# Attention and two feed-forward blocks on one core: two output places for lone heads, and the orders of small loads, exponentials, turns and fill pairs

## The reference, cut to what matters

```python
scores = scale * q @ k.T                       # (B, H, 576, 576)
cum = np.cumsum(np.maximum(s, 0), axis=-1)
bias = -(cum[..., :, None] - cum[..., None, :])
scores = np.where(causal, -1e9, scores + np.minimum(bias, 0.0))
scores -= scores.max(-1, keepdims=True)
attn = np.exp(scores); attn /= attn.sum(-1, keepdims=True) + 1e-9
x = heads_side_by_side(attn @ v)               # (B, 576, 512)
h = np.maximum(x @ w_in, 0)                    # 512 -> 1024
conv_out = conv over positions, 3 taps, per channel
x = (h * sigmoid(conv_out)) @ w_out            # 1024 -> 512
u = x + (x.T @ U @ V).T                        # mixes the 576 positions, rank 32
out = u + np.maximum(u @ w_ch1, 0) @ w_ch2     # 512 -> 2048 -> 512
```

## Time and profile before

| what | value |
|---|---|
| median of 3 runs | 921.22 us (920.56 to 921.58) |
| the profiled execution | 922.75 us |
| its span, first to last instruction | 921.0 us |
| PE busy | 873.2 us (95%) |
| DVE busy | 483.6 us (53%) |
| ACT busy | 373.2 us (41%) |
| POOL busy | 41.6 us (5%) |
| mean granted clock of TensorE | 0.98 |

### The profile page before, as it was taken

How to read it: one execution, slowest core, us unless ns; L and a number is a source line. 1 busy time by engine, 2 the same in 40 slices (tenths; PEclk the granted TensorE clock), 3 DMA queues, 4 the chain that set the end, 5 groups by cost and what they waited for, 6 DMA issues and landing times.

```text
span 921.0 us, 15633 instructions
## 1 busy us (share of the span) xinstructions
PE 873.2 (95%) x6184; PEld 831.9 (90%) x6184; DVE 483.6 (53%) x992; ACT 373.2 (41%) x709; POOL 41.6 (5%) x85
## 2 busy tenths in 40 slices
PE   4888898989999999999999999999999999999998
PEld 3676898879999999898999999988999999999998
DVE  6778794554448843554335871356225670442222
ACT  2667584654425634544233553444121431321110
POOL 3020000000000000000000000000000000000000
PEclk9979899989999999999999999999999999999999
DMA  7679356634764356435544453444243434355441
GB/s 161 167 211 308 111 149 204 217 79 149 239 200 173 131 190 200 153 115 198 174 153 144 144 170 113 166 128 163 92 151 140 181 138 177 144 189 182 145 177 52
DMA packets 63628, 149.14 MB, mean 162 GB/s; under 512 B 29514, under 2 KB 43850, under 8 KB 51012
## 3 DMA queue, kind: packets, MB, share of 16 engines
q1 hardware_dynamic: 61252, 144.50, 47.8%
q0 software_dynamic: 2304, 3.65, 1.7%
HBM read 117.97 MB, written 30.09 MB: 161 GB/s over the span
## 4 chain that ended last, share of the span: by engine, by line
PE 82%; DVE 8%; issue 4%; ACT 4%; DMA 1%; POOL 0%; DVEq 0%; ACTq 0%; POOLq 0%
PE psum L1170 22%; PE psum L1172 21%; PE psum L1171 21%; PE psum L1151 7%; PE psum L1098 3%; PE psum L1130 2%; PE psum L1128 2%; DVE psum L875 1%; PE psum L1135 1%; DVE work L942 1%; DMA spread_out<-few_scratch 1%; PE psum L1111 1%; ACT qc L675 1%; PE psum L1225 1%; DVE sums L895 1%
## 5 line engine op out<-in xcount | busy, mean ns | idle before, releaser
L1170 PE MATMUL psum<-uu_hl,ring 128*128 128x288 f32 x512 | 156.6, 306 | 7.6 <-DVE u_acc L997 2.9
L1170 PE MATMUL psum<-r_hl,ring 128*128 128x288 f32 x512 | 154.5, 302 | 1.9 <-DVE u_acc L997 1.1
L1172 PE MATMUL psum<-uu_hl,ring 128*128 128x288 f32 x512 | 152.8, 298 | 0.0
L1171 PE MATMUL psum<-uu_hl,ring 128*128 128x288 f32 x512 | 152.6, 298 | 0.0
L1172 PE MATMUL psum<-r_hl,ring 128*128 128x288 f32 x512 | 151.1, 295 | 0.0
L1171 PE MATMUL psum<-r_hl,ring 128*128 128x288 f32 x512 | 151.0, 295 | 0.0
L985 DVE SCALAR_TENSOR_TENSOR r_hl<-psum,r_hl 128x288 fp32r<-128x288 f32 x128 | 58.4, 457 | 133.9 <-ACT r_hl L773 133.9
L773 ACT ACTIVATE r_hl<-psum 128x288 fp32r<-128x288 f32 x128 | 52.4, 410 | 183.3 <-PE psum L1172 183.2
L1151 PE MATMUL psum<-probs,va 128*128 128x320 f32 (+4 forms) x448 | 117.4, 383 | 6.2 <-ACT probs L681 6.2
L875 DVE CUSTOM_DVE_ANT_0 psum<-psum,key_late 128x512 f32<-128x512 f32 (+4 forms) x160 | 84.7, 564 | 60.6 <-PE psum L1098 60.1
L1170 PEld LDWEIGHTS psum<-uu_hl,ring 128*128 128x128 f32 x512 | 97.8, 191 | 11.2 <-DVE u_acc L997 4.2
(11 more groups left out here) (104 smaller groups left out, 1654.1 us busy)
## 6 DMA issues: line engine op xcount, KB each, us to landing
ring<-w_scratch SPq DMA_DIRECT2D x74, 1024.0 KB, 4.8
w_scratch<-ring SPq DMA_DIRECT2D x24, 1024.0 KB, 6.1
kq_raw<-in_kq_t SPq DMA_DIRECT2D x64, 288.0 KB, 5.2
stage<-in_w_ch SPq DMA_DIRECT2D x16, 512.0 KB, 5.4
out_t<-u_acc SPq DMA_DIRECT2D x16, 288.0 KB, 3.9
va<-in_v SPq DMA_DIRECT2D x32, 128.0 KB, 2.4
spread_out<-few_scratch POOLq DMA_DIRECT2D x24, 144.0 KB, 4.3
stage<-in_w_out SPq DMA_DIRECT2D x4, 512.0 KB, 6.8
```

The lines of the kernel that those rows point to most:

```text
L1170: pe.matmul(o, hi, m_hi, start=start, stop=False)
L1171: pe.matmul(o, hi, m_lo, start=False, stop=False)
L1172: return pe.matmul(o, lo, m_hi, start=False, stop=stop)
```

## The change

- Output place: a head of body 0 with an even number gets its output four banks up (`out_at`), in banks 6 and 7; its values wait for the eviction of the head before the last one only. In body 0 the eviction of a head stands behind the next head's exponentials 0 and 1 on ACT (the last of the eight heads keeps its place).
- The small loads are issued in steps (0, 4), (1, 4) and (2, 2). POOL's memset writes the border columns of `hid` only, 4 instead of 1156.
- The turn stands in step 3 in all bodies; in bodies 1 to 3 it is behind the values of the step.
- `order`: the fill pair in the middle of "wi" goes, and where there are late pairs, one stands behind the split. With the spread by costs this moves other items by a step or two.
- ACT: after the last item of a step, the high part of a gated block and the making of a weight block (`follow`) stand behind the next attention step instead of ahead of it.
- DVE: x_low in bodies 1 to 3 stands behind the items of its step. `invert_few` of body 0 moves from step 3 to step 4.

```diff
@@ -224,6 +224,10 @@
         O0 = 3 * BANK - SPLIT
...
+        def out_at(n):
...
+            return O0 + 4 * BANK * (n < H and n % 2 == 0)
         MX = 4 * BANK
@@ -247,9 +251,10 @@
         UV_AT = (3, 2)
+        SMALL_AT = {(0, 4): 0, (1, 4): 1, (2, 2): 2}
         MAXIMA = [{0: (0, 1), 1: (2,)}, {0: (0,), 1: (1,), 2: (2,)}]
-        TURN = [3, 4]
+        TURN = [3, 3]
@@ -283,8 +288,6 @@
                 seq.extend(pair("wi", b, f))
-                if f == FT // 2:
-                    fill(1)
             fill(1)
@@ -298,12 +301,14 @@
                 fill_between(*([("mix", b, 0, d, half) for d in range(KT)] for half in range(2)))
+                seq.append(("split", b, 0, KT - 1, 0))
+                fill(1)
             else:
...
                     seq.extend(pair("mix", b, d))
-            seq.append(("split", b, 0, KT - 1, 0))
+                seq.append(("split", b, 0, KT - 1, 0))
             assert not late
@@ -427,6 +432,11 @@
+        LAST_OF_STEP = {items[-1] for plan in PLAN.values() for items in plan if items}
+        STEPS = [(a, h, g) for a in PLAN for h, g in ATT_STEPS]
+        STEP_BEFORE = dict(zip(STEPS[1:], [items for plan in PLAN.values() for items in plan]))
...
         X_SPLIT = [{(5, 0): 0, (7, 0): 1}, {(3, 4): 0, (5, 4): 1, (7, 4): 2}]
@@ -556,8 +566,8 @@
                     attention_step(0, h, g)
-                    if g == 4 and h < 3:
-                        load_small(h)
+                    if (h, g) in SMALL_AT:
+                        load_small(SMALL_AT[h, g])
                     if g == 1 and h - 1 in WEIGHTS_HEADS[:-1]:
@@ -640,7 +650,7 @@
                             pool.wait_ge(s_uvl, 2)
-                            pool.memset(hid[:, :, :], 0.0).then_inc(s_hid, 1)
+                            pool.memset(hid[:, :, 0:S + 2:S + 1], 0.0).then_inc(s_hid, 1)
@@ -683,6 +693,7 @@
                     o, sm = D * (h % 2), D * (1 - h % 2)
+                    out = out_at(n)
                     mm_pv.wait(act, n)
@@ -690,13 +701,13 @@
                     if h // 2 < NPAIR - 1:
-                        act.activation(sums[sm:sm + 1, h // 2 % 2, :], psf[sm:sm + 1, O0:O0 + S], ACT.Identity, bias=EPS)\
+                        act.activation(sums[sm:sm + 1, h // 2 % 2, :], psf[sm:sm + 1, out:out + S], ACT.Identity, bias=EPS)\
                            .then_inc(evict.sem, 1)
                     else:
-                        act.activation(sums[o:o + D, h // 2 % 2, :], psf[sm:sm + D, O0:O0 + S], ACT.Identity, bias=EPS)\
+                        act.activation(sums[o:o + D, h // 2 % 2, :], psf[sm:sm + D, out:out + S], ACT.Identity, bias=EPS)\
                            .then_inc(evict.sem, 1)
                     xl_done.wait(act, m - NPAIR)
-                    act.activation(x_raw[o:o + D, h // 2, :], psf[o:o + D, O0:O0 + S], ACT.Copy).then_inc(evict.sem, 1)
+                    act.activation(x_raw[o:o + D, h // 2, :], psf[o:o + D, out:out + S], ACT.Copy).then_inc(evict.sem, 1)
@@ -710,10 +721,12 @@
                         prepare_queries(a, h + 2)
-                    if g == 4:
+                    if g == 4 and (a or h == H - 1):
                         evict_head(a, h)
...
                         exponentials(a, h, c)
+                    if g == 0 and h and not a:
+                        evict_head(a, h - 1)
                     if (h, g) in X_SPLIT[a > 0]:
@@ -782,12 +795,26 @@
+                def follow(item):
+                    kind, b, unit, i, half = item
+                    if kind == "wi" and half and i:
+                        y_high(b, i - 1)
+                    for of, q in REFILL.get(item, ()):
+                        if made(of, q):
+                            weights_high(q)
...
+                def body_step(a, h, g):
+                    attention_step(a, h, g)
...
+                    if STEP_BEFORE.get((a, h, g)):
+                        follow(STEP_BEFORE[a, h, g][-1])
...
                 def ffn_step(item):
...
                         hidden(b, i, half)
-                        if i:
-                            y_high(b, i - 1) if half else gate(b, i - 1)
+                        if i and not half:
+                            gate(b, i - 1)
                     if kind == "gated":
@@ -800,9 +827,8 @@
                         hidden2(b, unit, i, half)
-                    for of, q in REFILL.get(item, ()):
-                        if made(of, q):
-                            weights_high(q)
+                    if item not in LAST_OF_STEP:
+                        follow(item)
@@ -813,7 +839,8 @@
                 act.wait_ge(s_hid, 1)
-                bodies(attention_step, ffn_step)
+                bodies(body_step, ffn_step)
+                follow(PLAN[B - 1][-1][-1])
                 for x, item in enumerate(END):
@@ -906,19 +933,19 @@
                         maxima(a, h + 1, r)
-                    if a and (h, g) in X_SPLIT[1]:
-                        x_low(a, X_SPLIT[1][h, g])
                     for pair in X_SPLIT_LAST[min(a, 2)].get((h, g), ()):
...
                         x_low(a, X_SPLIT[0][h, 0])
+                    if a and (h, g) in X_SPLIT[1]:
+                        x_low(a, X_SPLIT[1][h, g])
                     if g == 3 and not a:
...
                         query_low(a, h + 2)
-                    if g == 3 and h in (2, 4, 6):
+                    if g == 4 - (a > 0) and h in (2, 4, 6):
                         invert_few(a, h // 2 - 1)
@@ -1142,13 +1169,14 @@
                         v_in[i].wait(pe, a * NPAIR + h // 2)
-                        evict.wait(pe, n - 1)
+                        evict.wait(pe, max(n - 2, -1) if n < H else n - 1)
+                    out = out_at(n)
                     at = WIDTH[c]
...
                         first = (c, t) in ((0, 1), (3, 0))
-                        mm = pe.matmul(psf[:, O0 + i0:O0 + i1], va[i][:, t, :], probs[:, c % 2, at:at + w],
+                        mm = pe.matmul(psf[:, out + i0:out + i1], va[i][:, t, :], probs[:, c % 2, at:at + w],
                                        start=first, stop=True, skip_group_check=True)
@@ -1156,10 +1184,12 @@
                         scores(a, h, 1)
-                    if g == TURN[a > 0]:
+                    if g == TURN[0] and not a:
                         max_transpose(a, h + 1)
...
                         values(a, h, g - 1)
+                    if g == TURN[1] and a:
+                        max_transpose(a, h + 1)
                     if g in (1, 2):
```

## The result

The changed kernel takes **914.73 us** (median of 8 runs, 912.62 to 916.73) beside 921.31 us for the kernel before on the same chip (8 runs, 916.50 to 923.58): a ratio of 0.9934, 95% interval 0.9912 to 0.9956. It is faster, but by 6.6 us, where the sum had 17.7, and it lies above the upper end of the range, 913.

The account below looks back on a forecast made before the run. TensorE, busy 873.2 of 921.0 us, was taken as the bound, so only its idle and low-clock time could be won. Terms summed to -17.7 us: 903.5 on the median's scale, forecast 904, 8-in-10 range 898 to 913.

Parts of the forecast that it names:

- Lone heads, 0: Body 0's heads: PE's 0.42 us wait for exponentials only moves to DVE, so 0 us; bounds 2.9 won, 0.4 lost.
- Small loads, -5.0: Body 0 near 48 us: sooner small loads and a shorter memset end PE's stall and low clock, -5.0 us.
- rival 3: Small loads land no sooner, behind SP's queue and a 1 MB store: 909 us; chance 0.08.
- Transition, +0.5: Start of body 1: PE idles 3.4 us ahead of the sooner turn, products follow at low clock; +0.5 us.
- Body 1, gated part, +1.0: Exponentials' 2.37 us wait moves to DVE; low part and sooner turn wait some 0.65 us each; +1.0 us.
- Body 1, mixing part, -5.3: Waits of 1.57 and 1.64 us go, exponentials wait 1.5 us; idle -1.7, clock -3.6; bounds 0 and -6.1.
- So idle falls by 1.7: Body 1's mix: two waits go, about 1.5 us for exponentials comes instead, so 1.7 us less idle.
- stays up: Body 1's mix: full clock from 198.6 to 208.6 saves 4.4 us, less 0.8 us of wait: -3.6 us.
- Body 2, -3.8: Pair covers 1.9 us idle, low clock 1.7 and x_low's wait 1.2 go, gated part gives back 1.0: -3.8 us.
- Body 3, -5.1: Pair covers 1.9 us idle, low clock 3.0 and x_low's wait 1.2 go, gated part gives back 1.0: -5.1 us.
- The rule weighed in the prediction: Frequent small idles between groups of matmuls can also make the clock go down and up; by it rival 1 happens.
- rival 1: Several small waits stay in each mixing part and the clock falls all the same: 912 us; chance 0.20.

Follow-up runs that it names:

- one reordering by itself: Kernel before with nothing but x_low behind the step's items on DVE in bodies 1 to 3: 914.08 us, ratio 0.9913.
- the best kernel: Changed kernel with turn at step 4, y's high part at once, only the weights' high part behind the next attention step: 907.74 us, ratio 0.9846.

## Why the prediction was wrong, point by point

By the table (and with the 0.05 and 0.73 us of "up" counted to the mix) the parts changed as follows, from before to after:

| part | forecast | profile: idle + clock |
|---|---|---|
| body 0, up to the wait ahead of the turn | -5.0 | -1.95 + 1.6 = -0.35 |
| start and gated part of body 1 | +1.5 | +1.2 - 1.5 = -0.3 |
| mix of body 1 | -5.3 | +0.6 - 1.2 = -0.6 |
| body 2 | -3.8 | -0.1 - 1.7 = -1.8 |
| body 3 | -5.1 | -2.3 - 3.1 = -5.4 |

So two terms fell short by 4.7 us each, the small loads and the mix of body 1, and body 2 by 2.0. That the gated part does not show among them is the clock of this one execution and a shorter first wait; what it cost is told by the runs without turn and deferral.

**Lone heads, 0: right.** There the prediction followed the gain round the whole cycle of a head, to DVE; the terms that failed followed it one step.

**Small loads, -5.0: mis-sized**, 2 to 4 us where it shows, about 0 in the changed kernel. The step that failed is "Their four issues took 41.93 to 45.8, 3.9 us, so they end by 42.3": they began at 39.53, took 5.5 us and ended at 45.03. I counted the instructions that move, but put them behind a store and a load that are issued at 37.19 and 37.82, and gave them the durations they had had in another place. That is rival 3's mechanism, SyncE's queue and the 1 MB store ahead; its price was 5.0 us, as the term's. With the loads ahead of the store this step is mended and the time is still the same within the interval, so it is not all that the term had wrong: the next wait, for the spread sums, and the clock took the rest. The memset's part was right: the cast beside it takes 0.45 us instead of 1.40.

**Transition, +0.5: right in place.** The wait of 2.92 us gave way to one ahead of the turn, as said. It was forecast at 3.4 us; it was 1.50 us in after and 1.09 to 3.25 us in the other profiles with the sooner turn.

**Body 1, gated part, +1.0: two costs priced apart that are one.** "The 2.37 only moves there" was right about the place and wrong about the size: 3.06 us of waits became 5.67 (1.43, 1.43, 0.79, 2.02). The prediction had both pieces, the low part waiting where ACT copies now go first, and the turn meeting maxima just finishing, and priced each by itself at some 0.65 us. They are one chain: high part, low part, maxima, turn. With the deferral the low part waits 0.99 us at its head, and the turn at its end waits 1.43 us instead of 0.34. The runs with one or neither part show it: these waits (behind the first of the body, above 0.3 us) come to 2.9 us with the turn alone, 3.9 us with the deferral alone, 2.4 us with neither and 5.7 us with both.

**Body 1, mixing part, -5.3: the steps that failed are "So idle falls by 1.7" and "stays up".** The waits of 1.57 and 1.64 us went, but the idle time stayed: 5.12 + 0.05 us before, 5.08 + 0.73 after. "So idle falls by 1.7" took one successor, the exponentials at 1.5 us; four came, 1.49, 1.10, 1.20 and 0.73 (the last was in the sum, at 0.8). The clock gave 1.2 us of the 4.4 that were to come back. The ground for "stays up" was that 3.06 us of waits near 141 were followed by no low stretch, and this was one execution: nine of the eighteen profiles have that wait of 2.36 or 2.37 us, and in six of them the clock fell right behind it. The kernel before (its wait at 141.32), then the pair alone on it (its wait at 139.31):

```profile
140.00:150.00 10.00, 7.99 (x55) 7.41 (x56) 6.98 (x16) 5.55 (x10) 1.56 (x3) 1.00 0.78 240
```

```profile
140.00:150.00 10.00, 10.00 (x52) 9.47 (x51) 5.09 (x14) 3.43 (x7) 1.20 (x3) 0.66 0.55 195
```

The 0.69 us for maxima behind it stands in the three profiles whose clock stayed up and in none of the six. Without turn and deferral the idle time is 4.10 us, so x_low's order is worth 1.0 here; with the turn alone it is 5.09 us again, with the deferral alone 4.11, so it is the sooner turn that takes it back.

**Body 2, -3.8: half.** The pair's cover and the clock came (low 1.7 to 0). But with the pair behind the split two waits of 0.42 and 0.86 us for DVE stand at 400.09 and 408.66, in the mixing part; I had looked for what it gives back in the gated part. The 1.20 us wait at 381, which I laid on DVE's x_low, grew to 1.56. In after:

```profile
379.92 0.68 ACT L715 ACTIVATE x_hl<-x_raw 128x576 fp32r<-128x576 f32 x1 [1.36 <-DVE x_raw L916]
380.63 0.41 ACT L786 ACTIVATE r_hl<-psum 128x288 fp32r<-128x288 f32 x1
...
381.07 0.46 DVE L1012 SCALAR_TENSOR_TENSOR r_hl<-psum,r_hl 128x288 fp32r<-128x288 f32 x1 [0.40 <-ACT r_hl L786]
381.59 0.40 PE L1200 MATMUL psum<-uu_hl,ring 128*128 128x288 f32 x1 [1.56 <-DVE r_hl L1012]
```

DVE now waits for ACT's relu, and ACT stood 1.36 us for DVE's normalisation and then did x_high first. Moving x_low alone took 0.24 us off (0.96 in its own profile); the pair alone put 0.31 us on (1.51). I had moved one of two instructions that stand ahead of the eviction.

**Body 3, -5.1: right, by the sum.** Idle 5.08 to 2.82 and clock 3.1 to 0 make 5.4. But the 3.0 for the clock may be in part one execution's luck, since small loads alone have the old order there and lost nothing.

**The clock.** The sum priced the falls of one profile as sure. Their total was typical: over the 53 runs of the kernel before beside the experiments the mean granted clock is 0.981, which over the span makes 17.2 us, and over the 8 runs of after 0.988, 11.2 us. So most of the 6.6 us that the change gave is clock. With turn and deferral undone it is 0.988 too, so their 5.1 us are not. Where the falls stand is another matter. Of the eighteen profiles seventeen lost 3.2 to 5.1 us in body 1 from its mix on, one 1.5; the falls near 52 came and went, and those near 422 and 642 stood in one profile alone. The rule weighed in the prediction (the Trainium skill, TensorE: Matmul & The Clock Gate, section "A second HAM failure mode: psum-queue depth-cycling") is in line with body 1, where waits of 1.10 and 1.20 us are followed by a clock of 0.57 from 202 to 206 us. In bodies 2 and 3 the small waits of 0.42 and 0.86 us within the mixing part were followed by no fall (1.00 from 396 to 412 us and from 610 to 626), and behind the mixes no wait of PE is left. So rival 1, whose 912 was the nearest number, came in body 1 alone, where 3.6 of its 8.3 us were priced.

**Chances.** Faster was right. The range was too narrow since each rival was added to the forecast by itself, and parts of several came together: 3.6 us of rival 1, the 5.0 of rival 3 and 2.0 in body 2 on top of 904 make 914.6 (that this meets 914.7 so closely is luck in part, as the terms above scatter from one execution to the next). The rival that was missing is the one that decided: the change's own parts working against one another. Without turn and deferral the kernel takes 909.6 us, within the range.

## What to carry to other kernels

When a change both delays a producer and hurries its consumer, follow the chain between the two as one, over every engine, before pricing either; here each part alone cost 0.6 and 1.0 us by the medians and the two 5.1. Try the parts one by one: one reordering by itself gave as much as all of them, and the best kernel has four and a half of the six. A stretch of low clock in one profile is a sample; price it at how often it comes, from several profiles, and look at what a DMA's issue will stand behind, not only at how long it took where it was.

## What the runs showed of the hardware

I had not expected these:
- The two issues for U on SyncE took 0.58 and 0.52 us in an earlier portion, 0.58 and 1.05 us just ahead of a 1 MB store and a 512 KB load, 1.33 and 1.24 us in their old place, and 1.84 and 1.83 us just behind that store and load (1.86 and 2.35 us in the profile of small loads alone, 2.07 and 2.41 with x_low undone). The issue for V took 0.58 or 0.59 us in every place.
- The granted clock behind one and the same pair of waits (1.45 and 0.61 us) was 0.77 over 15 us in one execution and 1.00 in another, and behind one and the same wait of 2.37 us it fell in six executions and stayed up in three; nothing that I read in the traces decides it.
- The time of one kernel spread over 2 to 9 us from run to run (the kernel before 916.4 to 925.1 over the study). The granted clock accounts for a part of it: over the 53 runs of the kernel before it lay between 0.977 and 0.987, and the slower runs tend to be those with the lower clock (correlation 0.6 between the time and what the clock lost, some 0.5 us of time for 1 us lost). Where the rest comes from was not tested.
